# Batch mixing on one core: waits at part changes split by tile, products reordered, second weights in five loads

## The reference, cut to what matters

```python
# stage 1, recurrence (per batch and head, 768 steps)
y[t] = r[t] @ state
Sa = state @ a[t]
state = state * w[t] - outer(Sa, b[t]) + outer(v[t], k[t])
# stage 2, mixing (x is y with the heads side by side, 768 x 320)
h = x.T @ U @ V                       # U 768 x 32, V 32 x 768
u = x + h.T
x2 = u + relu(u @ w_ch1) @ w_ch2      # w_ch1 320 x 1280, w_ch2 1280 x 320
# stage 3, attention per expert e (4 of width 64), top 2 of 4 by x2 @ w_gate
q, k, v = x2 @ wq[e], x2 @ wk[e], x2 @ wv[e]
out += gate[:, e] * (softmax(causal(q @ k.T / 8)) @ v @ wo[e])
```

## Time and profile before

| | us |
|---|---|
| time, median of 3 executions (1179.33 to 1182.5) | 1180.62 |
| the profiled execution's own time | 1185.66 |
| its span, first to last instruction | 1183.8 |
| PE busy / PEld busy | 1042.8 / 775.8 |
| DVE / ACT / POOL busy | 539.9 / 397.3 / 324.5 |

### The profile page before, as it was taken

The page is one execution under the profiler, slowest core; times in us unless marked ns, Lnnn a source line. Parts: engine busy times, 40 slices in busy tenths (PEclk is TensorE's granted clock), DMA queues, the critical chain, the costliest instruction groups (busy, mean ns, idle before and its releaser), DMA issues. The chain is left out here.

```text
span 1183.8 us, 53706 instructions
## 1 busy us (share of the span) xinstructions
PE 1042.8 (88%) x24432; PEld 775.8 (66%) x24432; DVE 539.9 (46%) x1152; ACT 397.3 (34%) x1069; POOL 324.5 (27%) x588
## 2 busy tenths in 40 slices
PE   4767787899999997899999898799999898899878
PEld 4666677766676776666766686666666676555456
DVE  5544444343335875233433875423334875110274
ACT  2333333322123554322222464322112454310155
POOL 4544445332223432122322442112222420000000
PEclk9998988899999999899999998999999998999979
DMA  6232322413211221112211222102111111000000
GB/s 201 66 91 69 95 85 82 128 53 86 67 61 43 84 78 56 43 39 60 64 40 47 79 76 61 55 24 64 39 44 43 44 53 33 25 1 1 1 12 23
DMA packets 47937, 68.52 MB, mean 58 GB/s; under 512 B 19680, under 2 KB 34784, under 8 KB 47712
## 3 DMA queue, kind: packets, MB, share of 16 engines
q1 hardware_dynamic: 47712, 65.08, 18.5%
HBM read 57.19 MB, written 7.86 MB: 55 GB/s over the span
## 5 line engine op out<-in xcount | busy, mean ns | idle before, releaser
L486 POOL TENSOR_TENSOR QI<-R,consts 128x256 f32<-128x256 f32 x240 | 173.6, 733 | 467.0 <-DVE R L654 427.9
L654 DVE COPY R<-PB 128x512 f32<-128x512 f32 x147 | 100.6, 685 | 175.8 <-PE PB L912 173.7
L548 ACT COPY R<-PB 128x512 f32<-128x512 f32 x147 | 86.3, 587 | 220.9 <-PE PB L912 219.1
L904 PEld LDWEIGHTS PB<-R 64*64 64x64 f32 x5376 | 97.6, 139 | 68.9 <-issue 53.8
L904 PE MATMUL PB<-R 64*64 64x64 f32 x5376 | 117.8, 229 | 23.4 <-issue 8.2
L1137 PE MATMUL PB<-uf,W 128*128 128x384 f32 x320 | 111.5, 495 | 1.4 <-ACT ur L598 1.4
L1164 PE MATMUL PB<-work,W 128*128 128x384 f32 x320 | 107.4, 489 | 2.5 <-DVE work L829 2.5
L1137 PEld LDWEIGHTS PB<-uf,W 128*128 128x128 f32 x320 | 58.0, 190 | 46.5 <-issue 12.8
L912 PE MATMUL PB<-R,QI 64*64 64x64 f32 x3072 | 77.1, 223 | 11.3 <-issue 10.9
L1164 PEld LDWEIGHTS PB<-work,W 128*128 128x128 f32 x320 | 59.2, 190 | 41.8 <-issue 2.9
L829 DVE TENSOR_SCALAR work<-PB 128x384 f32<-128x384 f32 x40 | 22.3, 558 | 123.5 <-PE PB L1142 73.1
(11 more groups left out here) (136 smaller groups left out, 1903.5 us busy)
## 6 DMA issues: line engine op xcount, KB each, us to landing
EA<-ea_dram SPq DMA_DIRECT2D x48, 498.0 KB, 3.5
LA<-la_dram SPq DMA_DIRECT2D x48, 384.0 KB, 3.5
VT<-vt_dram SPq DMA_DIRECT2D x48, 80.0 KB, 1.9
x_mid_dram<-XO SPq DMA_DIRECT2D x192, 20.0 KB, 1.9
xs<-x_mid_dram SPq DMA_DIRECT2D x24, 160.0 KB, 3.0
out_dram<-work SPq DMA_DIRECT2D x24, 160.0 KB, 2.2
W<-w_dram SPq DMA_DIRECT2D x1, 1600.0 KB, 7.8
W<-w_dram SPq DMA_DIRECT2D x1, 1280.0 KB, 8.3
```

What stands on the lines that cost most here:

```text
L486: nc.gpsimd.tensor_tensor(QI[j][:].rearrange("p (u g t) -> p u g t", u=2, g=2), src.rearrange("p u (g t) -> p u g t", g=2), eye3.unsqueeze ...
L548: freed(nc.scalar.copy(tile[:, 8 * C:16 * C], PB[PLACE[group, i][0]][:, 1, :]), group, i)
L654: freed(nc.vector.tensor_copy(tile[:, 0:8 * C], PB[PLACE[group, i][0]][:, 0, :]), group, i)
L904: mm = nc.tensor.matmul(out[half(m1), u, col:col + C], left, right, start=True, stop=True)
```

## The change

In the mixing's list the u step of the 64 features left comes first, right behind z, and the four others are ordered by token half instead of by feature block. Within each u step the products with the identity come first and the product with z last, with the wait for z between them. The first h step waits for each u tile in front of the product that reads it, and for `("u", n, 2)` in front of the last two. x2_first waits for h 3 and h 4 only, and the wait for h 8 and h 9 moves to x2. The first v step waits for x2 `1, 0`, x2 `1, 1` and x2 `2` one after the other in front of the products that read them. Score 0 waits for the q and k of its own head pair, score 1 for those of the other. W2 is loaded by five transfers of 320 KB, issued as SP's loop comes to h 0, 2, 4, 6 and 8 of batch 0, and x2_first waits for all five; the attention's weights are issued at the first x2_first. The waits of `turn` are as before.

```diff
--- before.py
+++ after.py
@@ -82,7 +82,7 @@
 
 def mixing_steps(b):
 
-    mixing = ([("z", b)] + [("u", b, f, n) for f in range(2) for n in range(NH)] + [("u", b, 2)]
+    mixing = ([("z", b), ("u", b, 2)] + [("u", b, f, n) for n in range(NH) for f in range(2)]
               + [("h", b, m) for m in range(NM)]
               + [(what, b, f, n) for n in range(NH) for f in range(2) for what in ("x2_first", "x2")]
               + [("x2_first", b, 2), ("x2", b, 2)])
@@ -431,9 +431,11 @@
                     elif n == 1:
                         for m in range(2):
                             load_la(m)
-                elif (what, i, *args) == ("z", 0):
-                    sp.dma_start(W2[:], t["w2"].rearrange("(m p) n -> p m n", p=P)).then_inc(w2_in, 16)
-                elif (what, i, *args) == ("h", 0, NM - 1):
+                elif what == "h" and i == 0 and args[0] % 2 == 0:
+                    sp.dma_start(W2[:, args[0]:args[0] + 2, :],
+                                 t["w2"].rearrange("(m p) n -> p m n", p=P)[:, args[0]:args[0] + 2, :]
+                                 ).then_inc(w2_in, 16)
+                elif (what, i, *args) == ("x2_first", 0, 0, 0):
                     load_wide(WVG, "wvg", wvg_in)
                     load_wide(WK, "wk", wqk_in)
                     load_wide(WQ, "wq", wqk_in)
@@ -1096,37 +1098,31 @@
                     filled(mm, *step)
                 elif what == "u" and args[0] == 2:
                     b_ = turn(*step)
-                    is_out(pe, "z", n)
                     w = WID[2]
-                    for j in range(NH):
-                        nc.tensor.matmul(b_[j * w:(j + 1) * w, 0:HW], z[:, 2 * P:DM], Vw[:, j * HW:(j + 1) * HW],
-                                         start=True, stop=False, skip_group_check=True)
                     for i in range(HW // P):
                         for j in range(NH):
-                            mm = nc.tensor.matmul(b_[j * w:(j + 1) * w, i * P:(i + 1) * P],
-                                                  xs[:, j * (HW // P) + i, 2 * P:DM], ident, start=False,
-                                                  stop=(i == HW // P - 1), skip_group_check=True)
+                            nc.tensor.matmul(b_[j * w:(j + 1) * w, i * P:(i + 1) * P],
+                                             xs[:, j * (HW // P) + i, 2 * P:DM], ident, start=(i == 0), stop=False,
+                                             skip_group_check=True)
+                    is_out(pe, "z", n)
+                    for j in range(NH):
+                        mm = nc.tensor.matmul(b_[j * w:(j + 1) * w, 0:HW], z[:, 2 * P:DM], Vw[:, j * HW:(j + 1) * HW],
+                                              start=False, stop=True, skip_group_check=True)
                     filled(mm, *step)
                 elif what == "u":
                     b_ = turn(*step)
-                    is_out(pe, "z", n)
                     f, j = args
-                    nc.tensor.matmul(b_[:, 0:HW], z[:, f * P:(f + 1) * P], Vw[:, j * HW:(j + 1) * HW], start=True,
-                                     stop=False)
                     for i in range(HW // P):
-                        mm = nc.tensor.matmul(b_[:, i * P:(i + 1) * P], xs[:, j * (HW // P) + i, f * P:(f + 1) * P],
-                                              ident, start=False, stop=(i == HW // P - 1))
+                        nc.tensor.matmul(b_[:, i * P:(i + 1) * P], xs[:, j * (HW // P) + i, f * P:(f + 1) * P],
+                                         ident, start=(i == 0), stop=False, skip_group_check=True)
+                    mm = nc.tensor.matmul(b_[:, 0:HW], z[:, f * P:(f + 1) * P], Vw[:, j * HW:(j + 1) * HW],
+                                          start=False, stop=True, skip_group_check=True)
                     filled(mm, *step)
                 elif what == "h":
                     b_ = turn(*step)
                     m = args[0]
-                    if m == 0:
-                        for f in range(2):
-                            for j in range(NH):
-                                is_out(pe, "u", n, f, j)
-                        is_out(pe, "u", n, 2)
-                        if n == 0:
-                            pe.wait_ge(w1_in, 16 * 3)
+                    if (n, m) == (0, 0):
+                        pe.wait_ge(w1_in, 16 * 3)
                     lo = m * P
                     if m % 2:
                         for j in range(NH):
@@ -1134,9 +1130,13 @@
                                              stop=False, skip_group_check=True)
                     for j in range(NH):
                         for f in range(2):
+                            if m == 0:
+                                is_out(pe, "u", n, f, j)
                             mm = nc.tensor.matmul(b_[:, j, 0:HW], W1[:, f, lo:lo + P], uf[:, f, j * HW:(j + 1) * HW],
                                                   start=(f == 0 and m % 2 == 0), stop=(f == 1 and m % 2 == 1),
                                                   skip_group_check=True)
+                    if m == 0:
+                        is_out(pe, "u", n, 2)
                     if m % 2 == 0:
                         for j in range(NH):
                             mm = nc.tensor.matmul(b_[:, j, 0:HW], W1[half(j), 2, lo:lo + P], ur[half(j), :],
@@ -1147,12 +1147,15 @@
                     if what == "x2_first":
                         b_ = turn(*step)
                         if f == 0:
+                            for m in range(NM // 2 - 2, NM // 2):
+                                is_out(pe, "h", n, m)
+                            if n == 0 and args[1] == 0:
+                                pe.wait_ge(w2_in, 16 * (NM // 2))
+                    else:
+                        b_ = bank(*step)
+                        if f == 0:
                             for m in range(NM - 2, NM):
                                 is_out(pe, "h", n, m)
-                            if n == 0 and args[1] == 0:
-                                pe.wait_ge(w2_in, 16)
-                    else:
-                        b_ = bank(*step)
                     for m in range(NM // 2) if what == "x2_first" else range(NM // 2, NM):
                         if f == 2:
                             for j in range(NH):
@@ -1169,16 +1172,17 @@
                 elif what == "v":
                     b_ = turn(*step)
                     s = args[0]
-                    if s == 0:
-                        is_out(pe, "x2", n, 1, 1)
-                        is_out(pe, "x2", n, 2)
-                        if n == 0:
-                            pe.wait_ge(wvg_in, 16 * 3)
+                    if (n, s) == (0, 0):
+                        pe.wait_ge(wvg_in, 16 * 3)
                     for j in range(2):
                         lo = (s + j * NT // 2) * P
+                        if s == 0:
+                            is_out(pe, "x2", n, 1, j)
                         for f in range(2):
                             nc.tensor.matmul(b_[:, j, 0:NV + E], uf[:, f, lo:lo + P], WVG[:, f, :], start=(f == 0),
                                              stop=False, skip_group_check=True)
+                    if s == 0:
+                        is_out(pe, "x2", n, 2)
                     for j in range(2):
                         mm = nc.tensor.matmul(b_[:, j, 0:NV + E], ur[half(j), s * P:(s + 1) * P], WVG[half(j), 2, :],
                                               start=False, stop=True, skip_group_check=True)
@@ -1207,10 +1211,9 @@
                     turn(*step)
                     v = args[0]
                     s, j = v // 2, v % 2
-                    if v == 0:
+                    if s == 0:
                         for w in range(2):
-                            for i in range(2):
-                                is_out(pe, "qk", n, w, i)
+                            is_out(pe, "qk", n, w, j)
                     w = (s + 1) * P
                     parts = 2 if v >= 8 else 1
                     wide = w // parts
```

## The result

| | before | after |
|---|---|---|
| median of 10 executions each, same chip, us | 1178.07 (1172.71 to 1182.50) | 1171.70 (1162.0 to 1180.0) |
| ratio, 95% interval | | 0.9928 [0.9899, 0.9958] |
| profiled execution: own time / span | 1185.66 / 1183.8 | 1171.18 / 1169.4 |

The changed kernel is faster. The ratios, and the medians of the kernel before that are compared from one comparison to the next, leave out executions that fell in a slower state, and a ratio is not the quotient of two medians (here 0.9946). Two more comparisons of the same two kernels gave 0.9977 [0.9939, 1.0014] and 0.9952 [0.9920, 0.9983].

What follows compares the result with a forecast made beforehand. PE's own program was taken to bound the mixing, idle only at a handful of waits. Seven of twelve places gain 6.22 us, less 0.5 and 0.3 of costs: 5.4 off 1180.62 gives 1175.2 us, range 1171.8 to 1179.4.

Steps and rivals of the forecast that it cites:

- z to u: Batch 0, first u behind z: the moved 64-feature identity products fill PE's idle time; gain 0.66 us (bounds 0.5 and 0.78).
- u to h: First h behind the last u: batch 3 gains 0.83 us; batch 0 keeps its 0.78 idle through the bank wait.
- h to x2: x2_first behind h 9: batches 1 and 3 gain 1.00 us each, 2.00 together; batch 0 keeps waiting.
- x2 to v: First v behind the last x2: batch 2 gains 0.91 us; batch 3 gains nothing, since its bank's last user is x2 2.
- qk to score: Score 0 behind the last q's drain: gain 0.97 us in batch 1, 0.85 in batch 3, nothing in 0 and 2.
- The costs: Taken off the gain: 0.5 us for array switches at the 64-feature u step in four batches, 0.3 for new waits.
- rival 2: All twelve wait places pay, the bank waits being already satisfied; 4.8 us more, 1170.4 us; chance 0.05.
- Given back: Rival: the recurrence's turn in batches 1 and 2 swallows their gain; 2.7 us left, 1177.9 us; chance 0.17.
- the starts of the four mixings: Sign that the gain lasts: these starts should move by 0, some 0.4, some 2.2 and some 2.9 us.
- All twelve pay: Rival: the five places expected to keep waiting gain too, 4.8 us with overlap, giving 1170.4 us; chance 0.05.
- The clock gives more: Rival: less idle time around batch 3's first scores keeps PE's clock up; five pieces of 0.5 us, 1172.7; chance 0.08.
- Slower by W2's pieces: Rival: W2's five loads each delay a PE instruction fetch by 1.6 us, 8 us in all, 1183.2 us; chance 0.05.

Runs made afterwards that it cites:

- fewer_waits: Kernel before, with each first h, x2_first, v and score waiting only for the last drains; ratio 1.0014 [0.9979, 1.0049] against the kernel before.
- before_again: The kernel before, unchanged, run again against itself; ratio 1.0028 [0.9989, 1.0067], span 1189.5 us.
- placed: Changed kernel with other PSUM banks for the mixing, so that all twelve waits can go; ratio 0.9924 [0.9890, 0.9958] against the kernel before.
- score_only: Kernel before with only the wait of score 0 split by head pair; ratio 0.9980 [0.9947, 1.0014] against the kernel before.
- w2_only: Kernel before with W2 loaded in five pieces and the later attention weights; ratio 0.9979 [0.9953, 1.0004] against the kernel before.
- w2_one: Changed kernel with W2 in a single load at z and the attention weights at h 9; ratio 0.9946 [0.9919, 0.9972] against the kernel before.

## Why the prediction was right and wrong

**Which places pay: right, all twelve.** The seven that were to go have no idle time left, the five that were to stay still have it. Gaps before and after, and the term of the prediction beside the difference:

```
                    before  after  gained  forecast
z to u     b0        1.05   0.36    0.69    0.66
u to h     b3        0.94   0.32    0.79*   0.83
h to x2    b1, b3    1.33   0.32    2.02    2.00
x2 to v    b2        1.24   0.42    0.82    0.91
qk to score b1       1.29   0.42    0.87    0.97
qk to score b3       1.44   0.41    1.03    0.85
sum                                 6.22    6.22
stay: h to x2 b0 1.33 to 1.14, v b3 1.24 to 1.15, score b0 1.29 to 1.13,
      score b2 1.29 to 1.14, u to h b0 1.05 to 1.10*
```

(* The last product of u had 128 columns and has 384 now, which takes 0.17 more from start to start; this is taken out in the 0.79, and in batch 0 makes the 0.05 more a gain of 0.12.) The term of score 0 in batch 3 was too low by 0.18 at its place, and by 0.13 for the third score: I had let DVE's chain take part of it back, but the third score starts 2.28 us behind the first now and 2.23 before, so 0.98 of the 1.03 reaches it.

**The costs: too high.** I took 0.8 us off. The switch behind the step of 64 features costs 0.2 in batches 1 and 2 (z to h 15.36 to 15.56 us, the shortest in three traces each, where no block end adds to it) and nothing in batch 0, where z to h fell by 0.81, the 0.69 and 0.12 above; in batch 3 the half clock hides it. New waits: the same gaps of 0.32 and 0.42 appear at every place that pays, so they cost nothing that shows. And the five places that stay got 0.19 + 0.09 + 0.16 + 0.15 + 0.12 = 0.7 us shorter, which the prediction didn't have at all; fewer separate waits (`fewer_waits`) are a cause for part of it at most. That makes some 6.2 - 0.4 + 0.7 = 6.5 us instead of 5.4. The mixings, three traces each, average 584.6 and 577.5, 7.0 less; where the remaining half us comes from isn't shown, since block ends and half clock move single mixings by over 1 us. The whole time gives 6.1 [3.9, 8.3], in which 5.4, 6.5 and 7.0 all lie.

**The step that failed: "nothing in the terms depends on the difference, so I subtract from it: 1180.62 − 5.4 = 1175.2 us".** The base was taken as known, with the 3.2 us spread of three executions as its error. Ten executions of the same kernel beside the changed one had a median of 1178.07, 2.5 lower; with the 1.0 by which the difference of the medians (6.4) exceeds 5.4, that is the 3.5 us of the miss. The three are among the ten; the seven others have a median of 1175.75. The medians of the kernel before in the other comparisons, each on another chip, were 1178.8, 1185.1, 1183.9, 1181.8 and 1173.3: they cover 11.9 us, while my range was 7.6 wide in all. On one chip, too, two sets of its executions had 1178.8 and 1183.7 (`before_again`). The range had nothing for this, and it left out the 1170.4 of rival 2, to which I had given a chance of 0.05. The gain was inside what the terms allowed; the range for the time wasn't wide enough for its base.

**The rivals.** *Given back:* false. The mixings of batches 1 and 2 kept what they gained, 2.09 and 1.43 in the first pair of traces, 1.4 and 1.2 on the average of three each (2.0 and 0.9 were forecast, less the costs), and so nothing was taken back inside them. Nor behind them: the four attentions together average 375.8 us before and 375.7 after. My sign for it, the starts of the four mixings, failed: beside the first, which came 6.2 us earlier by the recurrence alone, they came 1.4 and 2.2 later and 3.7 earlier instead of 0.4, 2.2 and 2.9 earlier. The attentions between took 3.2 and 2.9 us more and then 4.5 less, which goes with the half clock in them. That sign was badly chosen: it moves more by itself than by the change. *All twelve pay:* false here, and true of `placed`, where the five places gave 0.79 (z to h of batch 0) + 0.88 (its h steps) + 0.73 + 0.72 + 0.72 (the gaps of v and of two scores) = 3.8 us (4.8 was the price, of which 0.7 had already come by themselves) and the mixings 3.3 and 1.8 in all (576.9 to 573.6 and 575.1), block ends and clock included. *The clock gives more:* open. In the last attention the six traces with all the changed waits spent 6.8 us at half clock and nine with the old wait 10.2 to 17.1, which is 1.0 us on average and not the 2.5 that I gave it; but the kernels of `placed`, which wait still less, don't have it, so the reason that I named, the idle time at score, doesn't hold. I saw this pattern only in looking the traces over; `score_only` tested the one wait, and no run was made for all of them together. *Slower by W2's pieces:* false, h of batch 0 took 56.03 us after and 56.23 before, and in `w2_only` 56.23.

**The costs taken as nothing.** W2's split shows no effect either way: `w2_one` at 0.9946 and the changed kernel at 0.995. The reordering of u pays only together with the waits: alone it is 1.0007, because the idle time moves from behind z to in front of h. The forecast counted its gain by itself and never said so.

## What to carry to other kernels

A wait split by tile pays only if nothing else in front of the same product waits for the same drain: find the last user of the output bank first, and give the part that follows another bank. Judge a change of a few us by the same place in two traces, start to start, where 0.01 to 0.03 us are resolved, and not by two spans, which differ by 10 us for one kernel. For the time itself, take the base as uncertain as its medians are between comparisons and chips, not as three executions of one are.

## What the runs showed of the hardware

**Block ends of PE's instructions cost up to 2.5 us each.** PE stands still at the same record of each 256. In the kernel before it does so for over 0.2 us at 37 of the 50 block ends before z of batch 0, 43 us in sum, and at 18 of the 145 behind, 13 us (idle time without a releaser; a part of it may have other causes). The Trainium skill (Runtime: NRT & Kernel Launch, section Instruction fetch mechanics) has instructions refilled in blocks of 16 KiB, 256 instructions, and calls crossing a boundary "mostly hidden". The size agrees with the 16 KB transfers here. "Mostly hidden" holds for most ends in the mixing, whose products are long, and not for those of the table above, at 0.4 to 1.3 us, nor for most ends in the recurrence alone, whose products are short. Why an end at one place costs and at another doesn't wasn't settled.

**One execution's granted clock moves by itself.** The recurrence alone, with identical instructions, took from 211.8 us (`placed`) to 223.4 (`fewer_waits`) in the traces, with 0.86 to 0.96 of the full 2.4 GHz on average in the windows shown. A straight line through the executions of the kernel before, in each of the five other comparisons, falls by 0.2 to 0.3 us for each us less at half clock (1.2 GHz).

**Separate waits behind a blocking one cost 0.06 to 0.2 us at some places** (`fewer_waits`; the falls at the five places that stay are of the same size), at others nothing; what tells these places apart stays open.
